# The second unit's square, product and four decayed products move from GpSimd to VectorE

## The reference, cut to what matters

```python
mag = np.sqrt(a_re * a_re + a_im * a_im)
scale = np.minimum(mag, 0.999) / (mag + 1e-06)
a_re_n, a_im_n = (a_re * scale, a_im * scale)
for t in range(S):
    ar, ai = (a_re_n[:, :, t, :, None], a_im_n[:, :, t, :, None])
    new_re = ar * S_re - ai * S_im
    new_im = ar * S_im + ai * S_re
    kv = np.einsum('bhd,bhe->bhde', k[:, :, t], v[:, :, t])
    S_re, S_im = (new_re + kv, new_im)
    y[:, :, t] = np.einsum('bhd,bhde->bhe', q[:, :, t], S_re)
...
h = x @ w_in
g = np.where(h > 0.0, h, alpha * (np.exp(np.minimum(h, 0.0)) - 1.0))
x = g @ w_out
...
h = np.maximum(np.maximum(x @ w1, x @ w2), x @ w3)
return (h @ w_out).astype(np.float32)
```

## Time and profile before

| what | value |
|---|---|
| median of 3 runs | 906.73 us (906.69, 906.73, 909.32) |
| profiled execution, its own time | 907.62 us |
| its span, first to last instruction | 905.8 us |
| TensorE busy | 840.5 us, 93% |
| VectorE busy | 443.3 us, 49% |
| ScalarE busy | 489.2 us, 54% |
| GpSimd busy | 335.1 us, 37% |

### The profile page before, as it was taken

How to read it: one execution, slowest core, us unless ns; L and a number is a source line. 1 busy time by engine, 2 the same in 40 slices (tenths; PEclk the granted TensorE clock), 3 DMA queues, 4 the chain that set the end, 5 groups by cost and what they waited for, 6 DMA issues and landing times.

```text
span 905.8 us, 14185 instructions
## 1 busy us (share of the span) xinstructions
PE 840.5 (93%) x5584; PEld 715.7 (79%) x5584; DVE 443.3 (49%) x628; ACT 489.2 (54%) x731; POOL 335.1 (37%) x254
## 2 busy tenths in 40 slices
PE   0178889889999999999999999999999999999998
PEld 0168889878887888788888888888888888888886
DVE  6679886848585858585858332333212121212120
ACT  7779778585959595959595635642121121112121
POOL 1165734534444444444444413555222130313021
PEclk9998999999999999999999999999999999999999
DMA  7763262444344434443443425002020202000000
GB/s 298 191 199 120 66 203 80 153 133 133 108 124 126 141 108 124 128 140 108 125 140 92 125 96 202 0 19 104 1 70 1 70 1 70 0 35 1 24 13 35
DMA packets 70146, 88.43 MB, mean 98 GB/s; under 512 B 15296, under 2 KB 52672, under 8 KB 69568
## 3 DMA queue, kind: packets, MB, share of 16 engines
q1 hardware_dynamic: 70080, 87.53, 31.1%
HBM read 59.13 MB, written 28.39 MB: 97 GB/s over the span
## 4 chain that ended last, share of the span: by engine, by line
PE 59%; issue 0%; ACT 0%; DVE 0%
PE bank L1243 59%; PE bank L1258 0%; ACT osb L704 0%; DVE xl L947 0%
## 5 line engine op out<-in xcount | busy, mean ns | idle before, releaser
L593 POOL TENSOR_TENSOR gl<-ge,gh 128x512 fp32r<-128x512 f32 x96 | 131.3, 1368 | 190.4 <-ACT gh L704 190.4
L947 DVE TENSOR_TENSOR hm<-bank,hm 128x512 f32<-128x512 f32 x72 | 49.8, 692 | 225.0 <-PE bank L1243 223.2
L1243 PE MATMUL bank<-xh,wih 128*128 128x512 f32 (+1 forms) x336 | 125.7, 374 | 6.9 <-DVE ge L944 3.6
L944 DVE SCALAR_TENSOR_TENSOR ge<-ge,bank 128x512 f32<-128x512 f32 x96 | 65.7, 685 | 131.0 <-ACT ge L704 131.0
L1243 PE MATMUL bank<-xh,wah 128*128 128x512 f32 x324 | 126.0, 389 | 0.0
L1243 PE MATMUL bank<-xl,wah 128*128 128x512 f32 x324 | 126.0, 389 | 0.0
L1243 PE MATMUL bank<-xh,wal 128*128 128x512 f32 x324 | 126.0, 389 | 0.0
L1243 PE MATMUL bank<-gh,woh 128*128 128x512 f32 (+1 forms) x336 | 123.9, 369 | 0.1
L593 POOL TENSOR_TENSOR hl<-hm,hh 128x512 fp32r<-128x512 f32 x36 | 46.5, 1293 | 204.3 <-ACT hh L704 204.3
L1243 PE MATMUL bank<-xl,wih 128*128 128x512 f32 (+1 forms) x336 | 121.9, 363 | 0.0
L1243 PE MATMUL bank<-xh,wil 128*128 128x512 f32 (+1 forms) x336 | 121.9, 363 | 0.0
(11 more groups left out here) (86 smaller groups left out, 1566.8 us busy)
## 6 DMA issues: line engine op xcount, KB each, us to landing
q_cols<-qp SPq DMA_DIRECT2D x24, 384.0 KB, 3.0
k_cols<-kp SPq DMA_DIRECT2D x24, 384.0 KB, 3.0
qt<-q_cols SPq DMA_DIRECT2D x24, 384.0 KB, 4.0
kt<-k_cols SPq DMA_DIRECT2D x24, 384.0 KB, 3.9
vv<-in_v SPq DMA_DIRECT2D x12, 448.0 KB, 4.7
qd<-in_q SPq DMA_DIRECT2D x12, 384.0 KB, 4.3
kd<-in_k SPq DMA_DIRECT2D x12, 384.0 KB, 4.9
x_rows<-x2s SPq DMA_DIRECT2D x6, 768.0 KB, 4.8
```

The source lines that it names most:

```text
L593: return nc.gpsimd.tensor_tensor(dst, whole, high.bitcast(f32), ALU.subtract)
L944: return nc.vector.scalar_tensor_tensor(out=dst, in0=a, scalar=s, in1=b, op0=op0, op1=op1)
L947: return nc.vector.tensor_tensor(dst, a, b, op)
L1243: return nc.tensor.matmul(dst, lhsT, rhs, start=start, stop=stop)
```

## The change

In the second unit the square of `ai`, the product for the tangent and the four decayed products are issued by VectorE's functions instead of GpSimd's; GpSimd begins with the third unit. The condition in both blocks that asks whether a piece is one of the first unit's now takes in the second unit's steps as well. The semaphore helpers follow: `SOLO` is 3, the number of parts whose work VectorE does alone, and the thresholds of GpSimd's counters shrink accordingly. In the table `AT_SECOND` four steps move: `square_im` -37 to -39, `tangent` -28 to -30, `decayed_a` -28 to -21, `decayed_b` -27 to -17.

```diff
     AT_SECOND = {
-        "square": -39, "square_im": -37, "squared": -39, "root": -35, "denominator": -34, "inverse": -30, "log_decay": -31,
-        "signed": -27, "tangent": -28, "arctan": -29, "angle": -22, "scan_lam": -28, "center": -24, "exps": -27, "ends": -26,
-        "scan_phi": -22, "reduced": -18, "decayed_a": -28, "decayed_b": -27, "sines": -16, "rotate_q_a": -13, "rotate_k_a": -12,
+        "square": -39, "square_im": -39, "squared": -39, "root": -35, "denominator": -34, "inverse": -30, "log_decay": -31,
+        "signed": -27, "tangent": -30, "arctan": -29, "angle": -22, "scan_lam": -28, "center": -24, "exps": -27, "ends": -26,
+        "scan_phi": -22, "reduced": -18, "decayed_a": -21, "decayed_b": -17, "sines": -16, "rotate_q_a": -13, "rotate_k_a": -12,
...
+        SOLO = last_part(1) + 1
+
         def of_gate(eng, first, later, p):
-            if p < PAIR:
+            if p < SOLO:
                 eng.wait_ge(first, p + 1)
             else:
-                eng.wait_ge(later, p - 1)
+                eng.wait_ge(later, p - SOLO + 1)
...
-            if z < 2 * PAIR:
+            if z < 4 * PAIR:
                 eng.wait_ge(qkd1, z + 1)
             else:
-                eng.wait_ge(qkd, z - 2 * PAIR + 1)
+                eng.wait_ge(qkd, z - 4 * PAIR + 1)
...
                 def now_later(what):
-                    return now(what) and x != AT_FIRST[what] and x != AT_FIRST_B.get(what)
+                    return now(what) and x not in (AT_FIRST[what], AT_FIRST_B.get(what), STEPS + AT_SECOND[what])
...
                 if z == 2:
-                    act.wait_ge(tan, 1)
+                    act.wait_ge(tan1, SOLO)
...
                 def now_first(what):
-                    return x in (AT_FIRST[what], AT_FIRST_B.get(what))
+                    return x in (AT_FIRST[what], AT_FIRST_B.get(what), STEPS + AT_SECOND[what])
```

## The result

| | before | change |
|---|---|---|
| median | 906.75 us (22 runs, 904.97 to 909.32) | 910.68 us (22 runs, 908.16 to 914.12) |
| ratio | 1 | 1.0041, 95% interval 1.0032 to 1.0051 |
| profiled execution, span | 905.8 us | 911.4 us |

The account below looks back on a forecast made before the run. TensorE's long row of matmuls bounds the kernel; its start can move. 3.87 + 0.92 - 1.03 = 3.76 us later: profiled 907.62 + 3.8 = 911.4, median 910.5 us; own range 909.8 to 911.4, range asked for 906.3 to 911.5.

Parts of the forecast that it names:

- The square: Second unit's square, now behind VectorE's last rotation: starts at 29.34, its sum 0.72 us later.
- The product: Tangent's product on VectorE from 39.07: `arctan` at 40.30, `signed` at 41.61, 0.35 us earlier with the square counted.
- The meeting: GpSimd's first `wol` (46.87) just ahead of VectorE's second decayed product (46.91) holds it; row 0's mask 3.87 us later.
- rival 1: VectorE goes first, nothing is held: `rotate_q` of row 2 moves +0.46, 907.2 us, no measurable change; chance 0.26.
- The way to the rotation: From row 0's mask to row 2's `rotate_q`: 3.87 + 0.92 (row 3's decayed products) - 1.03 (first `wil`) = 3.76 us later.
- The block: From 60 us on all queues move as one, by as much as row 2's `rotate_q`, to the span's end.
- rival 3: TensorE's later waits catch up 1 us or more of the 3.8: 909.4 us or less, same by measure; chance 0.08.
- Rival 2: VectorE's lasting shift against GpSimd removes TensorE's 3.11 us loss at 110.50 behind `ge`: 904.1 us, 0.3% faster; chance 0.08.

Follow-up runs that it names:

- Run 5: The change with the four decayed products back on GpSimd, so only square and product are VectorE's: 906.31 us, ratio to before 0.9987.
- run 6: The kernel before with only the product moved to VectorE; square and decayed products stay GpSimd's: 905.72 us, ratio to before 0.9988.
- run 1: The change plus two one-column copies on ScalarE ahead of the first `woh`, to delay GpSimd's first `wol`: 907.18 us, ratio to before 1.0003.
- run 3: The change with ScalarE's first `woh` ahead of `end_gain`, so GpSimd asks during `qd`: 910.63 us, ratio to before 1.0045.
- Run 4: The change with square and product back on GpSimd; only the four decayed products are VectorE's: 910.30 us, ratio to before 1.0040.
- run 9: The change plus the ScalarE copies delaying GpSimd's first `wol`, and the first `wil` behind row 2's rotations: 907.04 us, ratio to before 1.0002.
- run 7: The kernel before with only the product on VectorE and the first `wil` behind row 2's rotations: 903.42 us, run again 903.35 us.
- run 8: The kernel before with only the first `wil` moved behind row 2's rotations: 905.36 us, ratio to before 0.9983.
- run 2: The change with GpSimd's first `wol` waiting for the second unit's `reduced`: 907.33 us, ratio to before 1.0007.

## Why the prediction was right

**The square.** Expected at 29.34 and 0.72 of delay for the sum; it started at 29.34, the sum at 30.40, 0.79 later. The 0.07 too little is the time from the end of an instruction to the next that waits for its semaphore, here 0.11.

**The product.** Started at 39.10 (39.07), `arctan` at 40.38 (40.30), `signed` at 41.64 (41.61). The gain to `signed` was 0.31 (0.35). Run 5 shows the sum of both alone. That the product's gain was largely spent on the square is the difference between runs 5 and 6: the mask at 46.51 and at 45.67. That is a reading of the traces; the times of the two runs don't show it.

**The meeting.** This was the term that carried the forecast: 46.87 against 46.91 expected, 46.89 against 46.93 measured. The step that could have failed, who goes first with 0.04 us between them, went as in the pair at 99.32 and 99.39. The hold was 3.25 beyond the usual 0.55 (3.30 expected). It was no safe forecast: the sum's own errors were as large as the 0.04, and one row at 0.07 stood for the order. What made it come out is that both times hung on the same step, as the text against rival 1 says; both were 0.02 late. Runs 1 and 3 show both sides of it: 0.15 behind, and the price is gone; 0.14 ahead, and it is the same. Run 4 has it without the square and the product. The rule that the prediction drew from the Trainium skill (SBUF — State Buffer, "Who interferes with whom"), that the shared pair is an exclusive lock and that the order of issue decides who blocks, is borne out by every one of these rows: 3.80 us for an instruction of 0.55 when GpSimd started first, 0.55 when it started second.

**The way to the rotation.** 3.87 + 0.92 - 1.03 = 3.76 expected, 3.91 measured: 3.85 at the copy to `st`, 0.07 more from there to row 3's products, 0.94 for them, 1.03 less for the first `wil` (1.75 as said), and 0.08 more between the mask of row 1 and the rotation. One step of this part was wrong, though it hardly shows in the sum: ScalarE's waits were put at no cost, as standing at the same places. Its sines wait for row 3's decayed `kd`, which GpSimd had made by 51.6 and VectorE makes only by 58.8. With the `cs` at 61.57 the rotation at 61.65 could not have come earlier, and in run 9 the same wait costs 0.49.

**The block.** The wait for `qt` was expected unchanged at 4.75, ending at 72.7; it was 5.47 and ended at 73.07: TensorE was done with its work ahead of it at 67.60, 0.33 earlier than a shift of 3.76 would have it, and the rotated k was 0.2 us longer on its way to memory. The later shifts are 4.02 at the wait for `kr` and then, with the slower clock, 5.55 at 116 and 5.6 at the end. So nothing of the shift was caught up, and rival 3 is out. The medians, 910.68 measured and 910.5 expected, agree better than the terms allow to claim; the interval of the ratio reaches from 2.9 to 4.6 us, and the profiled execution was put at 911.4 and took 913.17.

**Rival 1** was the kernel of run 1: it was put at 907.2, and run 1 gave 907.18, 0.1 above its own runs of before where 0.46 was forecast; the interval (0.9 below to 1.5 above) holds both. **Rival 2** did not come: TensorE's wait for `ge` is 3.09 in the change, and 3.1 to 3.3 in all thirteen traces. It could not have decided as put, either: its 904.1 is not below the 904.0 that the prediction calls faster; for that 3.2 us of the wait would have to go, more than all of its 3.11, and not 2.6.

## What to carry to other kernels

Work taken off GpSimd makes the next thing in its queue start earlier; before moving it, ask what that is, when its data is ready, and which instruction of VectorE with two SBUF inputs it will then meet. If a long GpSimd instruction that nobody needs soon can start just ahead of a short one on the critical path, make it wait: 0.28 us of delay was worth some 3.5 us here. Ask too who waits for the moved result: ScalarE's sines hung on row 3's decayed product. And try the part that gains (the product) alone: it took 1.1 us off, and in the bundle with the square and the decayed products that was invisible.

## What the runs showed that was not expected

TensorE's pace between 48 and 60 us differs from one execution to the next. Row 1's 16 matmuls of scores took 3.75 us in nine of the thirteen traces, that of before and both of the change among them, but 2.02 in those of runs 1, 3, 7 (the first) and 8. In the trace of before the granted clock reads 1.00 (2.4 GHz) from 48 to 60 us, at the slow pace; in the first of the change it reads 0.50 (1.2 GHz) for the same 3.75 us. So the matmuls' own lengths are the better witness here.

A third place divides the traces cleanly. In seven (before, both of the change, runs 4, 5, 6 and 9) TensorE waits 2.67 us for `xl` between 182 and 190 us, and the 10 us behind that have a granted clock of 0.83 and 58 matmuls; in the other six (runs 1, 2, 3, 8 and both of 7) it waits 1.4 us, and the 10 us have 1.00 and 71 matmuls. The executions of the six took no longer than the median of their kernel; those of the seven lay above it. It does not follow the held `kd`, since run 3 is among the six, and before and the change are alike in it, so that it has no part in the difference of their spans. What decides it is not shown. With the stretch at 0.76 these go some way to explain why runs of one kernel lie 4 to 6 us apart, while 0.04 us between two engines move the median by 3.5.

The kernel of run 7 is the fastest of all, 903.4 us against 906.7 to 907.1 of before and 910.7 of the change.
